# Attention banks laid out anew: products of 320 and 256 columns instead of 512 and 64, and one exponential per sign

## The chip, the core and the metric

The kernel runs on one core of a Trainium2 chip. The metric is the device time of one execution in microseconds (us). Of the core's engines five names occur below: PE is TensorE (its weight loads are listed as PEld), ACT is ScalarE, DVE is VectorE, POOL is GpSimd, and SP is the queue that issues most DMAs. PE writes its products to PSUM, which has banks of 512 float32 columns; the products of one instruction lie in one bank.

## What is computed

A linear attention with exponential features, then two feed-forward stages on its output. The change touches only the attention. In its terms (8 batches, 8 heads, 576 tokens, 64 values per head, 128 features):

```python
def phi(x):
    proj = np.einsum('bhsd,df->bhsf', x, w_phi)
    proj = proj - np.max(np.abs(proj), axis=-1, keepdims=True)
    return np.concatenate([np.exp(proj), np.exp(-proj)], axis=-1)
q_p, k_p = (phi(q), phi(k))
kv = np.einsum('bhsf,bhsd->bhfd', k_p, v)
z = np.sum(k_p, axis=2)
num = np.einsum('bhsf,bhfd->bhsd', q_p, kv)
den = np.einsum('bhsf,bhf->bhs', q_p, z)[..., None] + 1e-06
return (num / den).astype(np.float32)
```

The result x goes through a mixing with the previous token, products with w_k, w_v and w_r (stage 1, `y_scr` in HBM holds its result), and then through w_in, a convolution over 3 tokens, a gate and w_out (stage 2).

## The kernel before

**Staging.** `phase_1` does the attention and stage 1 of all 8 batches, `phase_2` does stage 2. In `phase_1` the attention of batch 0 runs first and alone (`first_attention_steps`), while the weights of stage 1 are loaded, rounded by ACT and their remainders taken by POOL (L560). After that, each `iteration(c)` mixes stage 1 of batch c with the attention of batch c+1: `fill` puts tiles of stage 1 (K, R, V; 288 columns each) between the steps of the attention, by the costs in `PE_NS` and `FILL_NS`. These lists give every engine its order; semaphores join the engines. Within an engine nothing overtakes in the program.

**Attention of one pair of heads.** Two heads share the 128 partitions: head 0 has rows 0 to 63 of q and k, head 1 has rows 64 to 127. There are 4 pairs in a batch, 32 in all. The steps of a pair, by their names in the lists:

- E (`features_and_keys`, L597): the tail of the keys (`k_tail`, 128 columns, all 128 rows), the features of the queries (`feature_chunk`, the products q_in,phi) and 8 tiles of keys (`key_tile`). Batch 0 has F (`features_only`, L618) and G (`keys_only`) in its place. Products of head 0 use the upper 64 rows of the array, those of head 1 the lower 64, and PE runs the two beside each other.
- QT (`part_maxima`): DVE turns the features of both heads (`q_turn`, L974) and takes maxima (`q_part`); M: PE turns the maxima, DVE spreads them (`max_blocks`).
- KV, then PICK: PE sums keys times values, then `subtract_maxima` adds the negative maxima onto the features (max_blocks,pick), and `turn_back` (L692) turns the sums that ACT has copied out (`kvt`, L850). ACT then takes the exponentials (`exp_q`, L843), with `copy_back` of the sums after the first of them.
- DEN (`sum_den`, one row per head and sign; `sum_den_wide` for two pairs of batch 0) and NUM (`attend`): the products q_exp,kvz. ACT copies both results out, and the denominators go through HBM.

**The banks.** The 576 columns of a head don't fit in a bank. `att_psum` gives the three banks. Before, head 0 begins at column 0: 512 of its columns lie in bank 0 and 64 in bank 1. Head 1 begins at column 960: 64 columns lie in bank 1 and 512 in bank 2. The tail of the keys and the turned maxima lie between them in bank 1. `CHUNKS` holds these pieces and each product of queries is made piece by piece. Three products of different rows of the array write to bank 1, so the semaphore `shared_bank` keeps them apart: each waits until the one before it has ended.

## Time and profile before

| what | value |
|---|---|
| median of 3 runs | 1280.31 us (1279.93 to 1280.62) |
| the profiled execution | 1280.67 us, of which its span is 1278.9 us |
| PE busy | 1261.5 us, 99% of the span |
| DVE busy | 825.9 us, 65% |
| ACT busy | 553.5 us, 43% |
| POOL busy | 142.9 us, 11% |
| granted clock of PE | 0.999 over the span (2.4 GHz) |

The profile shows one execution. Its span runs from the first to the last instruction; 1.8 us of the execution lie around it. Products overlap in PE's pipeline, so the durations of single products are longer than the time that each adds: what one adds is read from the distance of its start to the next start. A float32 product is listed as two instructions with one weight load each, called passes below; the rounded ones (xy_hi, max_blocks and the like) are one.

### The profile page before, as it was taken

What the parts mean: (1) busy time and instruction counts of PE and PEld (TensorE: products, weight loads), DVE (VectorE), ACT (ScalarE), POOL (GpSimd) and SP (SyncE); (2) the same over time, 40 slices, a digit from 0 to 9 for tenths busy, and PEclk for the clock granted to TensorE, in tenths of its full rate; (3) what the DMA queues carried; (4) which work ended last, traced back from release to release, by engine and by line L of the source; (5) the groups of instructions that cost most, each with busy time, mean ns of one, the idle gap of its engine ahead of it and who ended that gap; (6) DMA issues with size and microseconds to landing.
All of it is one profiled execution on the core that took longest, in us unless ns stands there. A gap on an engine that the chain in (4) does not pass through costs nothing.

```text
span 1278.9 us, 23739 instructions
## 1 busy us (share of the span) xinstructions
PE 1261.5 (99%) x9548; PEld 1081.1 (85%) x9548; DVE 825.9 (65%) x1350; ACT 553.5 (43%) x1059; POOL 142.9 (11%) x137
## 2 busy tenths in 40 slices
PE   8899999999999999999999999999999999999998
PEld 6678797888788878888788878999889898898997
DVE  7888666676476666757656666546584593673863
ACT  4653543535435354353442544454343352352441
POOL 3412111211111211121111211000000000000000
PEclk9999999999999999999999999999999999999999
DMA  6512222221312212221131120421102102022001
GB/s 185 170 31 65 56 59 66 57 65 40 89 40 60 74 46 59 74 63 51 41 89 49 51 79 17 146 63 59 70 1 79 57 15 78 1 71 79 1 34 42
DMA packets 91700, 79.03 MB, mean 62 GB/s; under 512 B 61896, under 2 KB 70472, under 8 KB 90568
## 3 DMA queue, kind: packets, MB, share of 16 engines
q1 hardware_dynamic: 91432, 77.46, 20.0%
q8 instruction: 76, 1.25, 0.4%
q14 instruction: 32, 0.26, 0.1%
q10 hardware_dynamic: 160, 0.07, 0.0%
HBM read 58.21 MB, written 19.01 MB: 60 GB/s over the span
## 4 chain that ended last, share of the span: by engine, by line
PE 89%; DVE 4%; issue 3%; DMA 2%; ACT 2%; SPq 0%; ACTq 0%; DVEq 0%
PE psm L580 36%; PE ps L580 20%; PE psh L1221 6%; PE psh L1222 6%; PE psh L1220 6%; PE pso L1222 5%; PE pso L1221 5%; PE pso L1220 5%; DMA den<-den_scr 1%; ACT k_signs L832 1%; DMA den_scr<-den_cols 1%; PE ps L692 1%; DVE q_turn L974 1%; DVE q_part L977 0%; DMA phi<-in_w_phi 0%
## 5 line engine op out<-in xcount | busy, mean ns | idle before, releaser
L580 PE MATMUL psm<-xy_hi,wk_hi 128*128 128x288 f32 x512 | 156.5, 306 | 4.9 <-ACT relu L884 3.2
L580 PE MATMUL psm<-k_hi,wv_hi 128*128 128x288 f32 x512 | 153.8, 300 | 0.0
L1222 PE MATMUL psh<-xy_hi,win_lo 128*128 128x288 f32 x512 | 151.3, 296 | 0.0
L1220 PE MATMUL psh<-xy_hi,win_hi 128*128 128x288 f32 x512 | 151.3, 296 | 0.0
L1221 PE MATMUL psh<-xy_lo,win_hi 128*128 128x288 f32 x512 | 151.3, 296 | 0.0
L580 PE MATMUL psm<-xy_lo,wk_hi 128*128 128x288 f32 x512 | 151.1, 295 | 0.0
L580 PE MATMUL psm<-k_lo,wv_hi 128*128 128x288 f32 x512 | 150.9, 295 | 0.0
L580 PE MATMUL psm<-k_hi,wv_lo 128*128 128x288 f32 x512 | 150.8, 295 | 0.0
L580 PE MATMUL psm<-xy_hi,wk_lo 128*128 128x288 f32 x512 | 150.7, 294 | 0.0
L568 POOL TENSOR_TENSOR z_pairs<-k_signs 128x512 f32<-128x512 f32 x56 | 73.2, 1306 | 601.0 <-ACT k_signs L832 597.0
L1066 DVE TENSOR_TENSOR k_lo<-square,k_hi 128x288 fp32r<-128x288 f32 x128 | 76.6, 620 | 63.8 <-ACT square L889 63.0
L832 ACT ACTIVATE k_signs<-k_signs 128x1152 f32<-128x1152 f32 x32 | 37.2, 1163 | 156.0 <-issue 140.0
L580 PEld LDWEIGHTS psm<-xy_hi,wk_hi 128*128 128x128 f32 x512 | 96.1, 188 | 9.5 <-ACT relu L884 5.4
L1222 PE MATMUL pso<-wk_hi,g_lo 128*128 128x512 f32 x256 | 101.3, 396 | 0.0
L1220 PE MATMUL pso<-wk_hi,g_hi 128*128 128x512 f32 x256 | 101.3, 396 | 0.0
L1221 PE MATMUL pso<-wk_lo,g_hi 128*128 128x512 f32 x256 | 101.2, 395 | 0.0
L580 PE MATMUL ps<-q_exp,kvz 128*64 128x512 f32 (+2 forms) x960 | 98.4, 409 | 0.0
L580 PEld LDWEIGHTS psm<-k_hi,wv_hi 128*128 128x128 f32 x512 | 96.2, 188 | 1.8
L1221 PEld LDWEIGHTS psh<-xy_lo,win_hi 128*128 128x128 f32 x512 | 96.3, 188 | 0.3
L1220 PEld LDWEIGHTS psh<-xy_hi,win_hi 128*128 128x128 f32 x512 | 96.2, 188 | 0.3
L580 PEld LDWEIGHTS psm<-xy_lo,wk_hi 128*128 128x128 f32 x512 | 96.3, 188 | 0.0
L580 PEld LDWEIGHTS psm<-xy_hi,wk_lo 128*128 128x128 f32 x512 | 96.3, 188 | 0.0
(151 smaller groups left out, 2791.3 us busy)
## 6 DMA issues: line engine op xcount, KB each, us to landing
k_in<-in_k SPq DMA_DIRECT2D x32, 320.0 KB, 3.3
v_nat<-in_v SPq DMA_DIRECT2D x32, 320.0 KB, 3.5
q_in<-in_q SPq DMA_DIRECT2D x32, 288.0 KB, 3.1
y_scr<-y SPq DMA_DIRECT2D x64, 144.0 KB, 2.4
y<-y_scr SPq DMA_DIRECT2D x8, 1152.0 KB, 5.6
den<-den_scr SPq DMA_DIRECT2D x60, 144.0 KB, 3.0
out<-rows SPq DMA_DIRECT2D x32, 256.0 KB, 2.0
stage<-in_moe_w_in SPq DMA_DIRECT2D x4, 512.0 KB, 3.9
```

What stands on the lines that cost most here:

```text
L568: nc.gpsimd.tensor_tensor(z_pairs[:], tiles[:, 0], tiles[:, 1], ALU.add).then_inc(z_paired, 1)
L580: return nc.tensor.matmul(o, lhsT, rhs, start=first, stop=last, skip_group_check=True)
L692: last = nc.tensor.matmul(sums_back()[:, i, :], kvt[:, i, :], ident[:], start=True, stop=True, is_transpose=True, skip_group_check=True)
L832: nc.scalar.activation(k_exp, k_shift, ACT.Exp).then_inc(k_exp_ready, 1)
L974: nc.vector.transpose(q_turn[:, h, :], q_cols(h, p, a)).then_inc(q_turned, 1)
L1066: nc.vector.tensor_tensor(k2_lo[:, i, :], square[:, i % 2, :], k2_hi[:, i, :].bitcast(F32), ALU.subtract).then_inc(k2_lo_ready, 1)
L1220: nc.tensor.matmul(o, wh, xh, start=first, stop=False, skip_group_check=True)
L1221: nc.tensor.matmul(o, wh, xl, start=False, stop=False, skip_group_check=True)
L1222: return nc.tensor.matmul(o, wl, xh, start=False, stop=last, skip_group_check=True)
```

## The change

The two heads lie side by side, from column 192 to column 1344 of the three banks. Head 0 has 320 columns in bank 0 and 256 in bank 1, head 1 has 256 in bank 1 and 320 in bank 2. The tail of the keys moves to the front of bank 0, and the turned maxima behind head 1. The bytes computed are the same; every piece of 512 or 64 columns becomes one of 320 or 256.

Since both heads are now one stretch of 1152 columns, `exp_q` takes one exponential for each sign (2 of 1152 columns for 4 of 576), and `part_maxima` has one turn of 1152 columns for 2 of 576. `q_exp_ready` counts 2 for each pair instead of 4.

E and F now share `project_queries`: tail of the keys, then the bank 2 piece of head 1 and the bank 1 piece of head 0, then the bank 0 piece of head 0, then the bank 1 piece of head 1. In E the 8 tiles of keys all follow behind; before, three of them stood between the pieces.

```diff
-    Q0, K_TAIL, Q_MAX, Q1 = 0, BANK + D, BANK + D + 2 * F, 2 * BANK - D
-    CHUNKS = (((0, BANK), (BANK, S)), ((0, D), (D, S)))
+    HEAD_PART = BANK // 2
+    K_TAIL, Q0, Q1, Q_MAX = 0, BANK + HEAD_PART - S, BANK + HEAD_PART, BANK + HEAD_PART + S
+    CHUNKS = (((0, S - HEAD_PART), (S - HEAD_PART, S)), ((0, HEAD_PART), (HEAD_PART, S)))
...
+    def both_heads(p, a):
+        return att_psum(p, a)[:, Q0:Q0 + 2 * S].rearrange("p (h s) -> p h s", h=2)
...
+        def project_queries(p, a):
+
+            mm(k_tail(p, a), k_in[:, p % 2, P * (TT - 1):P * TT], phi[:], True, True).then_inc(shared_bank, 1)
+            feature_chunk(p, a, 1, 1, True)
+            feature_chunk(p, a, 0, 1, True).then_inc(shared_bank, 1)
+            await_(pe, shared_bank, 2 * PAIRS, a, 2 * p + 1)
+            feature_chunk(p, a, 0, 0, True)
+            await_(pe, shared_bank, 2 * PAIRS, a, 2 * p + 2)
+            feature_chunk(p, a, 1, 0, False).then_inc(raw_features, 1)
...
-            mm(k_tail(p, a), k_in[:, p % 2, P * (TT - 1):P * TT], phi[:], True, True).then_inc(shared_bank, 1)
-            feature_chunk(p, a, 1, 1, True)
-            feature_chunk(p, a, 0, 0, True)
-            key_tile(p, 1, 0)
-            await_(pe, shared_bank, 2 * PAIRS, a, 2 * p + 1)
-            feature_chunk(p, a, 0, 1, True).then_inc(shared_bank, 1)
-            key_tile(p, 1, 1)
-            key_tile(p, 0, 0)
-            await_(pe, shared_bank, 2 * PAIRS, a, 2 * p + 2)
-            feature_chunk(p, a, 1, 0, False).then_inc(raw_features, 1)
-            for h, t in ((0, 1), (1, 2), (0, 2), (1, 3), (0, 3)):
-                last = key_tile(p, h, t)
+            project_queries(p, a)
+            for t in range(TT - 1):
+                for h in (0, 1):
+                    last = key_tile(p, h, t)
...
-            for h in range(2):
-                for e in range(2):
-                    nc.scalar.activation(q_exp[:, e, h, :], q_cols(h, p, a), ACT.Exp, scale=1.0 - 2.0 * e).then_inc(q_exp_ready, 1)
-                    if a and h == e == 0:
-                        copy_back(p, a)
+            for e in range(2):
+                nc.scalar.activation(q_exp[:, e, :, :], both_heads(p, a), ACT.Exp, scale=1.0 - 2.0 * e).then_inc(q_exp_ready, 1)
+                if a and e == 0:
+                    copy_back(p, a)
...
-            for h in range(2):
-                nc.vector.transpose(q_turn[:, h, :], q_cols(h, p, a)).then_inc(q_turned, 1)
+            nc.vector.transpose(q_turn[:].rearrange("p h s -> p (h s)"), att_psum(p, a)[:, Q0:Q0 + 2 * S]).then_inc(q_turned, 1)
```

PE, the step E of a pair in the mixed iterations. In the program's order before (ps<-q_in,phi are the features, ps<-phi,k_in of the first row is the tail of the keys, the others are tiles of keys):

```order
L580 MATMUL ps<-phi,k_in 128x128 [waits q_loaded0,z_copied,k_loaded0,kvz_copied,num_copied]
L580 MATMUL ps<-q_in,phi 128x512 x2
L580 MATMUL ps<-phi,k_in 128x128
L580 MATMUL ps<-q_in,phi 128x64 [waits shared_bank]
L580 MATMUL ps<-phi,k_in 128x128 x2
L580 MATMUL ps<-q_in,phi 128x64 [waits shared_bank]
L580 MATMUL ps<-phi,k_in 128x128 x5
```

And now:

```order
L584 MATMUL ps<-phi,k_in 128x128 [waits q_loaded0,z_copied,k_loaded0,kvz_copied,num_copied]
L584 MATMUL ps<-q_in,phi 128x320
L584 MATMUL ps<-q_in,phi 128x256
L584 MATMUL ps<-q_in,phi 128x320 [waits shared_bank]
L584 MATMUL ps<-q_in,phi 128x256 [waits shared_bank]
L584 MATMUL ps<-phi,k_in 128x128 x8
```

The three tiles of keys that stood ahead of the last wait for `shared_bank` have moved behind it; one product of 320 columns stands there instead.

ACT, the step PICK of a pair in the mixed iterations, before:

```order
L850 ACTIVATE kvt<-ps 128x384 [waits kv_turned,kv_summed]
L843 ACTIVATE q_exp<-ps 128x576 [waits attended,features]
L855 ACTIVATE kvz<-ps 128x4x64 [waits attended,kv_turned]
L856 ACTIVATE kvz<-ps 128x4
L843 ACTIVATE q_exp<-ps 128x576 x3
L884 ACTIVATE relu<-psm 128x288 [waits k_squared,k_done]
```

And now:

```order
L849 ACTIVATE kvt<-ps 128x384 [waits kv_turned,kv_summed]
L842 ACTIVATE q_exp<-ps 128x1152 [waits attended,features]
L854 ACTIVATE kvz<-ps 128x4x64 [waits attended,kv_turned]
L855 ACTIVATE kvz<-ps 128x4
L842 ACTIVATE q_exp<-ps 128x1152
L883 ACTIVATE relu<-psm 128x288 [waits k_squared,k_done]
```

The copies of the sums (kvz) stand behind an exponential of 1152 columns instead of one of 576, and one exponential instead of three stands behind them. Nothing else changes its place.

## Rows read from the trace of the kernel before

**Rows 1.** The page: the span, and the chain that ended last by engine.
```profile
span 1278.9 us, 23739 instructions
...
PE 89%; DVE 4%; issue 3%; DMA 2%; ACT 2%; SPq 0%; ACTq 0%; DVEq 0%
```

**Rows 2.** Busy us (xinstructions) per engine: batch 0's attention, then the mixed iterations.
```profile
0.00:67.20 67.20, 57.59 (x454) 41.69 (x454) 53.02 (x77) 35.17 (x50) 26.27 (x25) 1.00 0.56 169
67.20:808.00 740.80, 736.72 (x6216) 610.83 (x6217) 487.59 (x851) 328.19 (x701) 116.62 (x112) 1.00 0.21 58
```

**Rows 3.** Timeline (start us, us, engine), step E of one pair, PE.
```profile
619.82 0.33 PE L580 MATMUL ps<-q_in,phi 64*128 64x64 f32 x2
...
620.27 0.32 PE L580 MATMUL ps<-q_in,phi 64*128 64x64 f32 x1
```

**Rows 4.** Timeline, the same step E, PE's weight loads.
```profile
618.85 0.30 PEld L580 LDWEIGHTS ps<-q_in,phi 64*128 64x128 f32 x4
...
620.26 0.18 PEld L580 LDWEIGHTS ps<-q_in,phi 64*128 64x128 f32 x1
...
620.37 0.19 PEld L580 LDWEIGHTS ps<-q_in,phi 64*128 64x128 f32 x1
...
621.13 0.19 PEld L580 LDWEIGHTS psm<-xy_hi,wr_hi 128*128 128x128 f32 x1
```

**Rows 5.** Timeline, a step F of batch 0, PE's weight loads.
```profile
28.92 0.30 PEld L580 LDWEIGHTS ps<-q_in,phi 64*128 64x128 f32 x4
29.46 0.19 PEld L580 LDWEIGHTS ps<-q_in,phi 64*128 64x128 f32 x1 [0.24 <-issue]
29.89 0.19 PEld L580 LDWEIGHTS ps<-q_in,phi 64*128 64x128 f32 x1 [0.24 <-issue]
30.27 0.29 PEld L580 LDWEIGHTS ps<-q_in,phi 64*128 64x128 f32 x2 [0.19 <-PE ps L580]
30.63 0.41 PEld L580 LDWEIGHTS ps<-v_nat,k_signs 128*128 128x128 f32 x3
```

**Rows 6.** Timeline, step PICK of one pair, PE's weight loads.
```profile
609.26 0.64 PEld L580 LDWEIGHTS ps<-max_blocks,pick 128*128 128x128 f32 x4 [0.22 <-issue]
609.95 0.36 PEld L692 LDWEIGHTS ps<-ident,kvt 128*128 128x128 f32 x3
```

**Rows 7.** Timeline, step PICK of another pair, PE's weight loads.
```profile
105.19 0.64 PEld L580 LDWEIGHTS ps<-max_blocks,pick 128*128 128x128 f32 x4 [0.72 <-DVE max_blocks L993]
105.77 0.46 PEld L692 LDWEIGHTS ps<-ident,kvt 128*128 128x128 f32 x3
```

**Rows 8.** Timeline, ACT in the step PICK of Rows 6.
```profile
609.40 0.49 ACT L850 ACTIVATE kvt<-ps 128x384 f32<-128x384 f32 x1 [1.67 <-PE ps L580]
...
611.12 1.76 ACT L843 ACTIVATE q_exp<-ps 128x576 f32<-128x576 f32 x3
612.72 0.47 ACT L884 ACTIVATE relu<-psm 128x288 f32<-128x288 f32 x1
```

**Rows 9.** Timeline, ACT, an exponential of 1152 columns of the keys.
```profile
599.80 1.17 ACT L836 ACTIVATE k_signs<-k_signs 128x1152 f32<-128x1152 f32 x1
600.88 0.39 ACT L884 ACTIVATE relu<-psm 128x288 f32<-128x288 f32 x1
```

**Rows 10.** Timeline, steps DEN and NUM of one pair, PE's weight loads.
```profile
613.67 0.22 PEld L580 LDWEIGHTS ps<-q_exp,kvz 128*1 128x1 f32 x16 [0.17 <-issue]
...
616.52 0.26 PEld L580 LDWEIGHTS ps<-q_exp,kvz 128*64 128x64 f32 x6 [0.28 <-issue]
616.85 0.19 PEld L580 LDWEIGHTS psm<-xy_hi,wr_hi 128*128 128x128 f32 x1
```

**Rows 11.** Timeline, DVE, both turns of one pair.
```profile
598.44 1.44 DVE L974 STREAM_TRANSPOSE q_turn<-ps 128x576 f32<-128x576 f32 x2
```

**Rows 12.** Timeline of batch 0's attention, DVE.
```profile
32.22 1.35 DVE L977 TENSOR_REDUCE q_part<-q_turn 128x36 f32<-128x1152 f32 x1
33.61 0.85 DVE L981 COPY q_part<-q_part 128x64 f32<-128x64 f32 x1
```

**Rows 13.** The same stretch, POOL.
```profile
31.99 2.42 POOL L560 TENSOR_TENSOR wv_lo<-mix,wv_hi 128x1024 fp32r<-128x1024 f32 x1
```

**Rows 14.** Timeline, PE, the first tile of stage 1.
```profile
67.28 0.37 PE L580 MATMUL psm<-xy_hi,wk_hi 128*128 128x288 f32 x1 [1.20 <-DVE xy_lo L1061]
```

More of the change, by code:

```diff
@@ L622, in features_only @@
             await_(pe, k_loaded[p % 2], 16 * (PAIRS // 2), a, 16 * (p // 2 + 1))
-            mm(k_tail(p, a), k_in[:, p % 2, P * (TT - 1):P * TT], phi[:], True, True).then_inc(shared_bank, 1)
-            feature_chunk(p, a, 1, 1, True)
-            feature_chunk(p, a, 0, 0, True)
-            await_(pe, shared_bank, 2 * PAIRS, a, 2 * p + 1)
-            feature_chunk(p, a, 0, 1, True).then_inc(shared_bank, 1)
-            await_(pe, shared_bank, 2 * PAIRS, a, 2 * p + 2)
-            feature_chunk(p, a, 1, 0, False).then_inc(raw_features, 1)
+            project_queries(p, a)
         def keys_only(p, a):
@@ L699, in sum_den @@
             await_(pe, z_copied, PAIRS, a - 1, p + 1)
-            await_(pe, q_exp_ready, 4 * PAIRS, a, 4 * p + 4)
+            await_(pe, q_exp_ready, 2 * PAIRS, a, 2 * p + 2)
             for chunk in CHUNKS[1]:
@@ L710, in sum_den_wide @@
             await_(pe, kvz_copied, PAIRS, a, p + 1)
-            await_(pe, q_exp_ready, 4 * PAIRS, a, 4 * p + 4)
+            await_(pe, q_exp_ready, 2 * PAIRS, a, 2 * p + 2)
             for chunk in CHUNKS[1]:
@@ L972, in part_maxima @@
             await_(dve, raw_features, PAIRS, a, p + 1)
-            for h in range(2):
-                nc.vector.transpose(q_turn[:, h, :], q_cols(h, p, a)).then_inc(q_turned, 1)
-            await_(dve, q_turned, 2 * PAIRS, a, 2 * p + 2)
+            nc.vector.transpose(q_turn[:].rearrange("p h s -> p (h s)"), att_psum(p, a)[:, Q0:Q0 + 2 * S]).then_inc(q_turned, 1)
+            await_(dve, q_turned, PAIRS, a, p + 1)
             await_(dve, max_turned, PAIRS, a, p)
```

## The prediction, made before the changed kernel was run

> **What bounds the kernel now.** I read the page first: the chain that ended last is PE for 89% of the span [rows 1]. Then the busy times by stretch [rows 2]. In the mixed iterations, 67.2 to 808 us, PE is busy 736.72 of 740.80 us, while DVE has 253 us of idle time, ACT 413 and POOL 624. Only the attention of batch 0 is different: PE is busy 57.59 of 67.20 us and DVE 53.02, so a chain through several engines sets the end there. In the mixed iterations, therefore, only what PE itself does in its order counts, and a faster DVE or ACT brings nothing unless PE waits for it. In batch 0 the latency of a pair counts. Stage 2 is not touched. Last I read PE's order in the three steps that the change touches, in the distances of starts. I looked at all pairs: the distances agree within 0.01 us, so one pair stands for all 28 mixed pairs (where one doesn't, I say so). All of it runs at the full granted clock, as the fields 1.00 of both stretches show.
>
> **Step E, features and keys.** From the first load of the queries (618.85) to the load of the next tile (621.13) it takes 2.28 us [rows 4]. Each half of the array (one head each) has its own work. A pass of 512 columns takes 0.43 us, the distance of two loads (29.46, 29.89) that each wait for the start of such a pass [rows 5]; I take other sizes in proportion, 0.27 for 320 and 0.21 for 256. A pass can't be shorter than a weight load, whose distance is 0.11 (620.26, 620.37) [rows 4], so a pass of 64 columns after a wait costs 0.11, and so does one of 128. Before, a half does 2 x 0.43, 2 x 0.11 and 8 x 0.11. After, it does 2 x 0.27, 2 x 0.21 and 8 x 0.11: 0.96 for 1.08, 0.12 less. But the wait has moved. The last piece (head 1, bank 1) waits until head 0's piece in bank 1 has ended. How long this takes is in step F: there the second pass of the short piece loads at 0.97 (29.89), is loaded at 1.08 and streamed at 1.13, and the waiting piece loads at 1.35 (30.27) [rows 5]: 0.22 from the last column to the release. Before, in E, tiles of keys ran in both halves during this wait. After, only one product of head 0 does, and head 1's half stands empty. The sum: head 1's first piece has streamed at 0.11 + 2 x 0.27 = 0.65, head 0's bank 1 piece at 0.11 + 2 x 0.21 = 0.53 to 0.54, so the last piece loads at 0.76, streams from 0.87 to 1.30, and 8 passes of keys follow to 2.18 or 2.19. With the change-over to a full array, 0.09 or 0.10 (1.13 + 0.11 to 30.63 leaves no more than that in F), the next tile loads at 2.28. Before: 2.28. **The shorter passes are lost to the wait; E costs 0.00 us.** The bounds are -0.03 and the rivals below. The features are ready some 0.4 us sooner than before (the last piece loads at 0.76, not 1.41), but DVE's large maxima still need the last tile of keys, which ends when it did.
>
> **Step PICK.** Four rounded products. After the first load, the fifth load (turn_back's) comes at 0.69 (609.26 to 609.95) [rows 6], and its product 0.11 later, at 0.80. Two of the four have 64 columns and cost a load of 0.11 each; that is where 256 columns would be free. The products before are 0.11 + 0.22 + 0.11 + 0.11 + 0.22 = 0.77; now 0.11 + 0.14 + 0.12 + 0.12 + 0.14 = 0.63 (a rounded product takes half a float32 pass and some 0.01). That would be 0.14 less. But the fifth load waits for ACT's copy `kvt`, which ends at 609.40 + 0.49 = 609.89, 0.06 ahead of the load [rows 8]. That copy hangs on the step KV ahead of PICK and doesn't move. Where PICK itself came late, the fifth load came at 0.58 [rows 7]: there alone, once in 28 pairs, the copy covers nothing. **So 27 pairs gain 0.00 us, one gains 0.14.**
>
> **Steps DEN and NUM.** 3.18 us (613.67 to 616.85) [rows 10]. The loads here are short (1 or 64 columns), so 64-column passes are nearly as good as others: the last four steps of 64 columns and the change-over take 616.52 to 616.85, 0.33; without 0.09 for the change-over that is 0.06 a step, against 0.053 in proportion. The new pieces save this excess: **0.02 us a pair**.
>
> **ACT and DVE.** Three exponentials of 576 columns take 611.12 to 612.72, 0.53 us each [rows 8]; one of 1152 takes 599.80 to 600.88, 1.08 [rows 9]. Four times 0.53 is 2.13, twice 1.08 is 2.16: the merging brings nothing. The two new exponentials read PSUM, the row reads SBUF, so I keep 0.1 us on both sides. The copies kvz come 0.5 us later; DEN, which needs them, begins at 613.67 [rows 10], 0.95 us after ACT has gone on to its next tile at 612.72 [rows 8], so they stay hidden. DVE's two turns last 1.44 us together [rows 11]; a reduction of 1152 elements lasts 1.35 [rows 12], my value for one turn of as many: 0.1 less, hidden by DVE's idle time in the mixed iterations.
>
> The Trainium skill (ScalarE: Activation LUTs, What ACT_TABLE_LOAD costs) gives an ACTIVATE 186 ns and 0.833 ns for each element, of which 93 ns overlap. By that, four of 576 would take 2.29 us and two of 1152 2.11, 0.19 less for each pair; over the four pairs of batch 0 at most 0.8 us less. The rows of this case show 2.13 and 2.16, and I go by them.
>
> **Batch 0.** Each pair's chain has one turn (0.1 less) and one PICK (0.14 less, since no turn_back follows). Step F falls from 1.71 (28.92 to 30.63) [rows 5] to 1.40, 0.3 less. If all four pairs kept all of this, 4 x 0.24 + 0.3 = 1.3 us would go. But POOL takes much of it back: DVE's copy at 33.61, some 0.2 us long at its shortest, lasted 0.85 [rows 12] and ended with POOL's instruction, 31.99 + 2.42 = 34.41 [rows 13]. If DVE comes sooner, it waits longer for POOL. I followed the chain to the first tile, for which PE stands idle 1.20 us [rows 14], shifting each start: two of the pairs end in such a wait and keep 0.1, and 0.3 us is left at the end. Bounds: 1.3 less, and 0.5 more (a long DVE instruction that newly falls under one of POOL).
>
> **The sum**, against the profiled execution, 1280.67 us (span 1278.9 and 1.8 around it): 28 x (0.00 + 0.00 - 0.02) = -0.56, the one PICK -0.14, batch 0 -0.3: -1.0 us, 1279.7. The median of the runs is 0.36 lower than the profiled execution, so the forecast is **1279.3 us**, -0.08%. Its own bounds: 28 x -0.03 and the rest of batch 0 give 1277.5, no gain and 0.5 more in batch 0 give 1280.8.
>
> **Rivals.**
>
> *The release comes in order (17%).* Head 0's bank 1 piece follows head 1's bank 2 piece in the order. If its end counts only once the longer one has ended (0.65 and not 0.54), the last piece loads 0.10 later: 28 x 0.10 = 2.8 us, 1282.1. For it: in E the waiting load came at 1.41, in F at 1.35, though the short piece streamed at the same time; something beside that piece delayed it by 0.06. Against: in the earlier layout the orders of the two halves were always of the same length, so no row shows whether one half waits for the other. The Trainium skill (TensorE: Matmul & The Clock Gate, The mechanism) says that matmuls start and end in program order without exception; by this rule the time would be this rival's.
>
> *The slower side: the waiting load needs an empty array (15%).* In E before, the short piece's passes are listed until 619.82 + 0.33 = 620.15, and the waiting piece begins at 620.27 [rows 3], just when the tiles of keys in flight in both halves had ended. If that is the rule after a wait, the last piece can load only when head 0's bank 0 piece has streamed, at 0.54 + 2 x 0.27 = 1.08 and not at 0.76. Head 1's half then stands empty 0.32 us longer, on PE's own path in each of 28 pairs: +9.0 us, 1288.3. It outweighs all gains (1.0 us) as soon as the load is 0.04 us late. Against it: turn_back's load at 609.95 waited for ACT too and came while the last product of PICK, until about 610.03, was still streaming [rows 6].
>
> *PICK's gain survives (5%).* If the fifth load is set by something that moves with the products, 27 x 0.13 = 3.6 us go: 1275.7. Against it speaks that it came 0.10 sooner where the copy was early [rows 7].
>
> *Nothing moves (9%).* DVE meets POOL as before at each point of batch 0, and E rounds up: 1280.3.
>
> **Chances and range.** The forecast has 54%. The range 1277.5 to 1283.1 holds it, the release in order with its bounds, and the case in which nothing moves; it leaves out 20%. About 0.2% (2.6 us) is what a measurement of this kernel can tell from no change. Faster by more: PICK's gain (5%) and the lower edge of the forecast (3%), 8%. Slower by more: the empty array (15%) and the upper edge of the release in order (3%), 18%. Within: 74%.
>
> **What would show it.** E from the first load of the queries to the next tile: 2.28 (2.38 and 2.60 under the rivals), with the last piece's load at 0.76 (0.86, 1.08). PICK's fifth load at 0.69 after the first, with a gap ahead of it that was not there. DEN and NUM 3.16. Two exponentials at 1.08 each. The first tile of stage 1 at 67.0. I would be wrong if PE's stream in a half depended on the other half, or if DVE's turn of 1152 columns were slower than two of 576.

## The result, and the profile after

The changed kernel takes **1281.53 us** (median of 20 runs, 1280.16 to 1284.75) against 1279.32 us (20 runs, 1278.39 to 1282.03) for the kernel before: a ratio of 1.0017, 95% interval 1.0012 to 1.0023. It is 2.2 us slower, where 1.0 us less was forecast. (The forecast of 1279.3 was reckoned from a median of 3 runs, 1280.31; over 20 runs the kernel before has 1279.32.) Among the runs of bank1_first, bank1_first_key_ahead and m_late_warm, below, is one execution each of 1.7 to 4.3 ms; without it their medians move by less than 0.3 us. The profiled execution took 1282.21 us with a span of 1280.4 us.

The page has hardly moved: PE still carries 89% of the chain that ended last [rows 1].

```profile
span 1280.4 us, 23643 instructions
...
PE 89%; DVE 4%; issue 3%; ACT 2%; DMA 2%; POOL 0%; SPq 0%; ACTq 0%; DVEq 0%
```

Step E, PE's weight loads (start us, us), three stretches of the same pair as in [rows 4]: the first load, the loads around the last piece (620.25 to 621.12), and the next tile.

```profile
620.25 0.19 PEld L584 LDWEIGHTS ps<-q_in,phi 64*128 64x128 f32 x2
...
621.12 0.18 PEld L584 LDWEIGHTS ps<-q_in,phi 64*128 64x128 f32 x1
621.13 0.18 PEld L584 LDWEIGHTS ps<-phi,k_in 64*128 64x128 f32 x1
...
622.64 0.19 PEld L584 LDWEIGHTS psm<-xy_hi,wr_hi 128*128 128x128 f32 x1
```

E takes 2.39 us (620.25 to 622.64) for 2.28 before. Its last piece loads 0.87 or 0.88 after the first load; 0.76 was forecast. All 28 mixed pairs agree within 0.01 us.

PICK of the pair in [rows 6], PE's weight loads:

```profile
610.72 0.56 PEld L584 LDWEIGHTS ps<-max_blocks,pick 128*128 128x128 f32 x4 [0.22 <-issue]
611.40 0.31 PEld L692 LDWEIGHTS ps<-ident,kvt 128*128 128x128 f32 x3
611.68 0.19 PEld L584 LDWEIGHTS psm<-xy_hi,wk_hi 128*128 128x128 f32 x1
```

The fifth load comes 0.68 after the first, as before. But turn_back then lasts 0.28 us to the next tile (611.40 to 611.68), where it lasted 0.33 (609.95 to 610.28; the next tile before):

```profile
610.28 0.19 PEld L580 LDWEIGHTS psm<-xy_hi,wk_hi 128*128 128x128 f32 x1
```

ACT in the same step [rows 8], with the two long exponentials, 1.03 and 1.02 us from start to the next start:

```profile
610.86 0.49 ACT L849 ACTIVATE kvt<-ps 128x384 f32<-128x384 f32 x1 [1.67 <-PE ps L584]
611.55 1.13 ACT L842 ACTIVATE q_exp<-ps 128x1152 f32<-128x1152 f32 x1 [0.20 <-PE ps L584]
612.58 0.38 ACT L854 ACTIVATE kvz<-ps 128x256 f32<-128x256 f32 x1
...
612.89 1.15 ACT L842 ACTIVATE q_exp<-ps 128x1152 f32<-128x1152 f32 x1
613.91 0.44 ACT L883 ACTIVATE relu<-psm 128x288 f32<-128x288 f32 x1
```

DVE's one turn of 1152 columns starts at 599.91, and the reduction behind it at 601.31:

```profile
599.91 1.37 DVE L972 STREAM_TRANSPOSE q_turn<-ps 128x1152 f32<-128x1152 f32 x1
601.31 1.35 DVE L975 TENSOR_REDUCE q_part<-q_turn 128x36 f32<-128x1152 f32 x1
```

In batch 0, step F of [rows 5] takes 1.50 us (28.34 to 29.84) for 1.71:

```profile
28.34 1.17 PEld L584 LDWEIGHTS ps<-q_in,phi 64*128 64x128 f32 x8
29.84 0.30 PEld L584 LDWEIGHTS ps<-v_nat,k_signs 128*128 128x128 f32 x2 [0.33 <-issue]
```

And there the granted clock is not whole any more. Three stretches of batch 0 (us, PE busy, granted clock, DMA share, GB/s), and PE ahead of M of pair 3:

```profile
46.00:49.00 3.00, 0.58 (x9) 1.00 0.89 233
49.00:52.00 3.00, 3.00 (x17) 0.62 0.24 59
52.00:55.00 3.00, 3.00 (x21) 0.81 0.80 272
```

```profile
48.81 0.30 PE L646 MATMUL psm<-ident,q_part 128*128 128x128 f32 x1 [2.42 <-DVE k_signs L958]
```

PE was idle for 2.42 us, and then part of the next stretches ran at the lower level, 1.2 GHz. In the profile of before the clock is 1.00 throughout batch 0. The first tile of stage 1 starts at 68.14 us; it was 67.28 [rows 14]. Whether the clock costs this time is looked at under batch 0, below.

Where the 2.2 us are, by the traces: from the first E of the mixed iterations (91.29 before, 91.77 after) to the end of the span, stage 2 included, it takes 1187.6 us before and 1188.6 after. Two further traces of the same kernels (below) give 1187.4 and 1188.9. So some 1.2 us are lost in the mixed iterations, and about 1 us is left for batch 0. That rest is a difference of medians less a difference of traces: the first E alone differs by 1.5 us between two traces of one kernel (below).

### The profile page after: what moved, and what is told of

It reads as the page before. It is cut to its first block, busy times and chain, and to the rows that moved or that the text cites. A ratio compares the mean times of both kernels' runs of the same rounds, so it can differ in the third digit from the quotient of the medians.

```text
span 1280.4 us, 23643 instructions
## 1 busy us (share of the span) xinstructions
PE 1262.1 (99%) x9548; PEld 1098.6 (86%) x9548; DVE 825.7 (64%) x1318; ACT 551.2 (43%) x995; POOL 143.0 (11%) x137
## 4 chain that ended last, share of the span: by engine, by line
PE 89%; DVE 4%; issue 3%; ACT 2%; DMA 2%; POOL 0%; SPq 0%; ACTq 0%; DVEq 0%
PE psm L584 36%; PE ps L584 20%; PE psh L1219 6%; PE psh L1220 6%; PE psh L1218 6%; PE pso L1219 5%; PE pso L1218 5%; PE pso L1220 5%; PE ps L692 1%; ACT k_signs L832 1%; DVE q_turn L972 1%; DMA den<-den_scr 1%; DVE q_part L975 1%; DMA den_scr<-den_cols 1%; DMA phi<-in_w_phi 0%
## 5 line engine op out<-in xcount | busy, mean ns | idle before, releaser
L584 PE MATMUL ps<-q_exp,kvz 128*64 128x320 f32 (+2 forms) x960 | 99.8, 413 | 0.0
L584 PEld LDWEIGHTS psm<-k_lo,wv_hi 128*128 128x128 f32 x512 | 96.3, 188 | 0.0
```

What stands on the lines that cost most here:

```text
L584: return nc.tensor.matmul(o, lhsT, rhs, start=first, stop=last, skip_group_check=True)
```

## The experiments

Each kernel was timed beside the kernel before on the same chip, but not all on one chip: the groups can be told by the column "before" (1279.79, 1279.30, 1279.61, 1279.03). Between groups, compare the differences from the kernel before. Medians in us, E and the load of its last piece in us after the first load:

| kernel | median (lowest run, runs) | before | ratio (95%) | E | last piece |
|---|---|---|---|---|---|
| bank1_first | 1277.25 (1276.25, 12) | 1279.79 | 0.9982 (0.9968 to 0.9996) | 2.27 | 0.75 |
| bank1_first_key_ahead | 1271.50 (1270.77, 6) | 1279.79 | 0.9929 (0.9909 to 0.9950) | 2.06 | 0.76 |
| m_late | 1281.13 (1279.58, 12) | 1279.79 | 1.0009 (0.9995 to 1.0022) | 2.39 | 0.88 |
| layout_alone | 1280.98 (1280.17, 12) | 1279.79 | 1.0006 (0.9995 to 1.0017) | 2.39 | 0.88 |
| before_again | 1279.48 (1278.40, 11) | 1279.30 | 1.0003 (0.9994 to 1.0012) | 2.28 | 1.42 |
| after_again | 1281.55 (1280.12, 11) | 1279.30 | 1.0014 (1.0005 to 1.0023) | 2.39 | 0.88 |
| pick_extra | 1282.20 (1281.22, 9) | 1279.30 | 1.0027 (1.0018 to 1.0037) | 2.39 | 0.88 |
| keys_behind | 1290.18 (1288.88, 4) | 1279.30 | 1.0084 (1.0070 to 1.0098) | 2.66 | 1.35 |
| key_ahead | 1275.90 (1275.22, 9) | 1279.61 | 0.9965 (0.9950 to 0.9981) | 2.17 | 0.88 |
| all_best | 1271.15 (1270.86, 5) | 1279.61 | 0.9936 (0.9924 to 0.9948) | 2.06 | 0.76 |
| round_in_parts | 1282.29 (1280.24, 12) | 1279.61 | 1.0021 (1.0010 to 1.0032) | 2.39 | 0.88 |
| m_late_warm | 1279.99 (1278.74, 11) | 1279.03 | 1.0008 (0.9999 to 1.0017) | 2.39 | 0.88 |
| all_best_warm | 1273.43 (1270.02, 5) | 1279.03 | 0.9944 (0.9931 to 0.9958) | 2.06 | 0.76 |

### Step E: what releases the last piece

**bank1_first**: head 0's bank 1 piece goes ahead of head 1's longer one; nothing else moves.

```diff
+            feature_chunk(p, a, 0, 1, True).then_inc(shared_bank, 1)
             feature_chunk(p, a, 1, 1, True)
-            feature_chunk(p, a, 0, 1, True).then_inc(shared_bank, 1)
```

> The changed kernel with one exchange: head 0's piece in bank 1 is issued ahead of head 1's piece in bank 2. In the changed kernel the last piece of a step E loads 0.88 us after the first load, and E takes 2.39 us. Theory A, the release comes in the order of the products (the short piece counts as ended only when the longer one issued ahead of it has ended): now nothing longer is ahead of it, so the last piece loads at 0.76 to 0.78 and E takes 2.28 to 2.29; 29 steps x 0.10 = 2.9 us less than the changed kernel. Rival B, the last piece can load only when its own half of the array has drained (head 1's first piece, which takes as long as before): the load stays at 0.86 to 0.88 and E at 2.38 to 2.39, the time unchanged. Rival C, both halves must be empty: excluded already by 0.88, which lies ahead of the end of head 0's bank 0 piece at 1.07.

PE's weight loads, step E of the same pair: first load, last piece, next tile.

```profile
615.73 0.94 PEld L584 LDWEIGHTS ps<-q_in,phi 64*128 64x128 f32 x7
...
616.48 0.18 PEld L584 LDWEIGHTS ps<-q_in,phi 64*128 64x128 f32 x1
...
618.00 0.19 PEld L584 LDWEIGHTS psm<-xy_hi,wr_hi 128*128 128x128 f32 x1
```

The last piece loads at 0.75 instead of 0.88 and E is 2.27. The same products in the same halves, only their order differs: the release of the bank 1 piece had waited for the longer product issued ahead of it in the other half of the array. That this wait needs an empty half is refuted. The kernel is 4.3 us faster than the changed one (2.5 below its before, where the changed kernel is 2.2 above): 28 x 0.123 = 3.4 of it is E, the rest was not followed up.

**bank1_first_key_ahead** also puts one tile of keys of head 1 ahead of the last wait, so that head 1's half has work during it. **key_ahead** does this alone, without the exchange.

```diff
-        def project_queries(p, a):
+        def project_queries(p, a, ahead=()):
...
             feature_chunk(p, a, 0, 0, True)
+            for h, t in ahead:
+                key_tile(p, h, t)
             await_(pe, shared_bank, 2 * PAIRS, a, 2 * p + 2)
...
-            project_queries(p, a)
-            for t in range(TT - 1):
-                for h in (0, 1):
-                    last = key_tile(p, h, t)
+            project_queries(p, a, ((1, 0),))
+            for h, t in ((0, 0), (1, 1), (0, 1), (1, 2), (0, 2), (1, 3), (0, 3)):
+                last = key_tile(p, h, t)
```

> As bank1_first, and one tile of keys of head 1 (two passes of 0.11) stands ahead of the last wait, so that head 1's half has work until 0.86. If what E loses is the empty half of the array and nothing else (theory A and B alike), the passes now follow each other: 0.11 + 0.54 + 0.22 + 0.43 + 6 x 0.11 = 1.96, with the change-over 2.06 us for E against 2.39 in the changed kernel and 2.29 in the one before. That is 28 x 0.33 = 9 us less than the changed kernel and 28 x 0.27 = 7.5 us less than the kernel before with the gain in the step PICK: a ratio to the kernel before of about 0.994. If the shorter passes were no gain at all (rival: a pass of 256 or 320 columns costs more than in proportion), E would stay at 2.17 or more.

> The changed kernel with one tile of keys of head 1 ahead of the last wait of E; the order of the two short pieces stays as in the changed kernel. It tells whether the late release costs by itself or only because head 1's half stands empty during it. Theory one (the release comes in order, at 0.88 after the first load, and PE loses only what nothing fills): the last piece loads at 0.88 to 0.89, the tile's two passes lie ahead of it at 0.65 and 0.76, and E falls by two passes of 0.11 from 2.39 to 2.18; 28 x 0.21 = 6.0 us less than the changed kernel, 1275.5 us. Theory two (the tile ahead of the wait pushes the waiting piece back by its own length): last piece at 1.0 or later, E 2.3 to 2.4, 1279 to 1281.5 us.

With key_ahead the release is as late as in the changed kernel (0.88), but E falls by 0.22: two passes of 0.11 now lie under the wait. PE's weight loads: the first load, the last piece with a load of the other half beside it, and the next tile:

```profile
198.93 0.52 PEld L584 LDWEIGHTS ps<-q_in,phi 64*128 64x128 f32 x5
...
199.81 0.18 PEld L584 LDWEIGHTS ps<-q_in,phi 64*128 64x128 f32 x1
199.81 0.18 PEld L584 LDWEIGHTS ps<-phi,k_in 64*128 64x128 f32 x1
...
201.10 0.19 PEld L584 LDWEIGHTS psm<-xy_hi,wr_hi 128*128 128x128 f32 x1
```

So the late release costs only what stands empty meanwhile. 28 x 0.223 = 6.2 us were to go; 6.0 went (2.25 above its before in after_again, 3.71 below in key_ahead). Both cures together bring E to 2.06 and the kernel to 1271.50 us, as expected: 8.3 us below the kernel before.

**keys_behind** asks the same of the old layout: the kernel before with its three covering tiles moved behind the waits.

```diff
-            key_tile(p, 1, 0)
             await_(pe, shared_bank, 2 * PAIRS, a, 2 * p + 1)
             feature_chunk(p, a, 0, 1, True).then_inc(shared_bank, 1)
-            key_tile(p, 1, 1)
-            key_tile(p, 0, 0)
             await_(pe, shared_bank, 2 * PAIRS, a, 2 * p + 2)
             feature_chunk(p, a, 1, 0, False).then_inc(raw_features, 1)
-            for h, t in ((0, 1), (1, 2), (0, 2), (1, 3), (0, 3)):
+            for h, t in ((1, 0), (0, 0), (1, 1), (0, 1), (1, 2), (0, 2), (1, 3), (0, 3)):
```

> The kernel before, in its old layout with pieces of 512 and 64 columns, but with all 8 tiles of keys behind the last wait in E, as the changed kernel has them. It takes the cover of the wait away and leaves all lengths. Theory one (three tiles of keys filled the wait): E is then step F with 8 tiles behind it: the last piece loads at 1.35 after the first as in F, its two passes take 0.11 each, 8 passes of keys in each half 0.88, and the change-over 0.10: 2.55 instead of 2.28, 28 x 0.27 = 7.5 us more than before, 1287.1 us. Theory two (PE is bound by its total of passes in a half and the wait costs nothing wherever it stands): E stays at 2.28 and the time at 1279.6 us.

The last piece loads at 1.35, as in F, but E is 2.66 and not 2.55, because the expectation left out the 0.11 us in which the waiting piece's own weights are loaded into an empty half. 28 x 0.377 = 10.6 us; measured 10.7 (1290.18 less 1279.48). Without cover E takes 2.66 in the old layout and 2.39 in the new one: the new lengths save 0.27 and the cover of the old order was worth 0.38. This run also bears on the release: with no tile of keys issued ahead of the short piece, the last piece loads at 1.35 and not at 1.42.

### PICK: does ACT's copy cover it

**pick_extra** repeats one product of 256 columns in PICK.

```diff
-            for h in range(2):
-                for chunk in CHUNKS[h]:
+            for h, chunks in enumerate((CHUNKS[0], (CHUNKS[1][:1] if a else ()) + CHUNKS[1])):
+                for chunk in chunks:
```

> The changed kernel with one more product of 256 columns in PICK of the 28 mixed pairs (head 1's bank 1 piece has its maxima subtracted twice, so the output is another). It measures what cover ACT's copy of the sums gives. Theory one (the load of turn_back waits for that copy, as predicted): the fifth load of PICK stays at 0.68 after the first where PICK has PE waiting for the copy; where the copy is early it comes 0.12 to 0.14 later than 0.51. Turn_back follows products that have only just ended and gets back to 0.33 from 0.28, so a pair costs 0.05 to 0.08, 28 pairs 1.4 to 2.2 us, 1283.3 us. Theory two (the load is set by the products): it moves to 0.80, and the kernel takes 28 x 0.13 = 3.6 us longer, 1285.1 us.

PE's weight loads in one PICK:

```profile
187.90 0.68 PEld L584 LDWEIGHTS ps<-max_blocks,pick 128*128 128x128 f32 x5 [0.23 <-issue]
188.58 0.32 PEld L692 LDWEIGHTS ps<-ident,kvt 128*128 128x128 f32 x3
188.87 0.19 PEld L584 LDWEIGHTS psm<-xy_hi,wk_hi 128*128 128x128 f32 x1
```

With five products turn_back's load still comes at 0.68: the copy sets it, as predicted. But turn_back stays at 0.29, so the extra product costs 0.65 us in all (1282.20 less 1281.55), where 1.4 to 2.2 were expected; the traces show 0.01 in each of 27 pairs and 0.11 in the one that the copy doesn't cover. Turn_back is thus not slowed by how much ran ahead of it. What fits all three traces is that it waits for a product that is still streaming: its first product is listed 0.11 after its load before, where the last old product has 512 columns (610.06 after 609.95), and 0.07 after it here (188.65 after 188.58), where that has 320.

### The mergers on ACT and DVE

**layout_alone** keeps the new layout with four exponentials and two turns (q_exp_ready still counts 2).

```diff
-            for e in range(2):
-                nc.scalar.activation(q_exp[:, e, :, :], both_heads(p, a), ACT.Exp, scale=1.0 - 2.0 * e).then_inc(q_exp_ready, 1)
+            for h in range(2):
+                for e in range(2):
+                    done = nc.scalar.activation(q_exp[:, e, h, :], q_cols(h, p, a), ACT.Exp, scale=1.0 - 2.0 * e)
...
-            nc.vector.transpose(q_turn[:].rearrange("p h s -> p (h s)"), att_psum(p, a)[:, Q0:Q0 + 2 * S]).then_inc(q_turned, 1)
+            for h in range(2):
+                nc.vector.transpose(q_turn[:, h, :], q_cols(h, p, a)).then_inc(q_turned, 1)
```

> The changed kernel with both mergers undone: four exponentials of 576 columns and two turns of 576, in the new layout of the banks. If the mergers bring nothing in the mixed iterations (my step), all distances on PE from 90 us on stay as in the changed kernel within 0.01 us: E 2.39, PICK to turn_back 0.68, DEN and NUM 3.17, and an iteration of 105.5 us. In batch 0 each pair is 0.1 to 0.25 us slower. The time lies within 1 us of the changed kernel. Rival: the mergers are what slows it (the copies kvz come 0.5 us later behind the longer exponential); then this kernel is faster than the changed one by 1 us or more.

In the mixed iterations nothing differs (E 2.39, PICK 0.68, DEN and NUM 3.17), and the medians 1280.98 and 1281.53 can't be told apart by their intervals. ACT there:

```profile
611.64 1.76 ACT L843 ACTIVATE q_exp<-ps 128x576 f32<-128x576 f32 x3
613.23 0.47 ACT L886 ACTIVATE relu<-psm 128x288 f32<-128x288 f32 x1
```

The last three take 0.53 each, and the first took 0.55: 2.14 us against 2.05 of the merged ones. The 0.09 are hidden.

### Batch 0: meetings and the granted clock

**before_again** and **after_again** are the two kernels once more.

> The kernel before, unchanged, run once more to see how much of batch 0 differs from execution to execution. In the trace at hand its granted clock stays at 1.00 through batch 0, and the first step E of the mixed iterations begins at 91.29 us. Theory one (the changed kernel loses about 1 us in batch 0 because PE's longer idle stretch there brings the half clock): the clock stays at full here again, E of the first mixed pair begins at 91.3 +-0.2, and the median is 1279.3 to 1279.8 us. Theory two (the clock falls somewhere in batch 0 in any of the kernels, by chance of the execution): a stretch at half clock shows here too, and E begins later than 91.3 by up to 1.7 us.

> The changed kernel, unchanged, run once more beside the kernel before on the same chip. In the mixed iterations nothing should differ from its first trace: E 2.39, the fifth load of PICK at 0.68 and turn_back 0.28, so 1.0 us over the whole of them. Theory one (half clock behind the idle 2.42 us ahead of M of pair 3): again a stretch at half clock near 50 us, and the first mixed E at 91.8. Theory two (chance): the stretch lies elsewhere, has another length or is not there, and the first mixed E begins between 90.3 and 91.8; the median is then 1.0 to 2.2 us above before whichever it is. Median expected: 1281.5 +-0.5 us.

before_again keeps the full clock in batch 0; its first mixed E starts at 89.83, where theory one said 91.3: executions of one kernel differ by 1.5 us here. In after_again that E starts at 90.82, and the half clock lies elsewhere, behind an idle time of 0.94 us of PE ahead of M of pair 0, which was 0.52 in the kernel before. Rows of PE, busy and clock:

```profile
15.00:18.00 3.00, 2.87 (x20) 0.77 0.00 0
18.00:21.00 3.00, 3.00 (x21) 0.66 0.49 117
```

The mean granted clock that each run lists says how often this is so. Runs at 1.000: 77 of 101 for the kernel before, 7 of 31 for the changed kernel. Theory two has the place right (it varies), theory one the tendency. Two limits. A mean of 0.999 need not come from batch 0: the kernel before shows it in both its traces with a full clock there, because the clock also falls at the very end (us; busy us of PE, PEld, DVE, ACT and POOL; clock; DMA share; GB/s):

```profile
67.20:1270.00 1202.80, 1198.56 (x9050) 1034.24 (x9051) 772.47 (x1274) 517.54 (x1008) 116.62 (x112) 1.00 0.18 55
1270.00:1278.90 8.90, 5.36 (x46) 5.16 (x44) 0.41 (x1) 0.77 (x2) 0.00 (x0) 0.92 0.35 113
```

And the changed kernel's 7 runs at 1.000 have a median of 1281.16 us, its other 24 of 1281.77, while the 77 of the kernel before have 1279.41. So 1.75 of the 2.2 us are there at full clock too. That leaves some 0.5 us for the clock (an estimate, from 7 runs) and, of the about 1 us of batch 0, about as much for something else.

The old layout is not free of the fall either: in the trace of keys_behind PE idles 2.12 us ahead of M of pair 3, and the clock is at its lower level from 49.8 to 53.2.

**m_late** puts M of pair 3 behind NUM of pair 2 on PE in batch 0.

```diff
             if m is None:
+                late = ("M", PAIRS - 1)
+                steps = [s for s in steps if s != late]
+                steps.insert(steps.index(("NUM", PAIRS - 2)) + 1, late)
```

> The changed kernel with one exchange in PE's order in the attention of batch 0: the step M of pair 3 stands behind the steps DEN and NUM of pair 2, so that PE, which idled 2.4 us ahead of that M and then ran at the half clock for 3.4 us (DEN and NUM of pair 2 took 5.7 us and not 4.0), idles 1 us at most there. Theory D, a part of the slowdown is this fall of the clock: no half clock in the first 90 us, DEN and NUM of pair 2 at 4.0 to 4.1 us, the first tile of stage 1 about 1.5 to 2 us earlier than the 68.1 of the changed kernel, and the time 1 to 2 us below the changed kernel. Rival: the clock falls in few executions only and the slowdown lies in step E alone; then the time changes by less than 0.5 us.

The half clock near 50 us is gone (1.00 from 49 to 55), but one stands from 17 to 21 (0.86 for 15 to 18, 0.57 for 18 to 21). The median is 1.34 us above its before, where the changed kernel is 2.2 above: the intervals of the two ratios overlap.

**round_in_parts** splits one rounding of ACT into 8 instructions, to let POOL begin later.

```diff
-            nc.scalar.activation(hi[:, i:i + rows, :].rearrange("p r n -> p (r n)"), stage[n % 3], ACT.Copy).then_inc(piece_hi, 1)
+            parts = 8 if n == 6 else 1
+            for j in range(parts):
+                cols = slice(1024 // parts * j, 1024 // parts * (j + 1))
+                nc.scalar.activation(hi[:, i:i + rows, :].rearrange("p r n -> p (r n)")[:, cols], stage[n % 3][:, cols], ACT.Copy).then_inc(piece_hi, 1)
...
-            pool.wait_ge(piece_hi, n + 1)
+            pool.wait_ge(piece_hi, n + 1 + 7 * (n >= 6))
```

> The changed kernel, with one rounding of ACT in batch 0 (the seventh piece of the weights, 1024 columns, done from 40.45 to 41.5 us) made in 8 instructions of 128 columns. That takes about 1 us longer and lets POOL begin its subtraction of this piece at about 42.6 us instead of 41.6. Nothing else changes. Theory one (batch 0 of the changed kernel loses time because DVE's multiplication x of 576 columns, at 42.07 us, meets this subtraction of POOL and lasts 2.5 to 2.9 us instead of 0.76): x comes ahead of POOL and lasts 0.76, the turn of pair 3 begins at about 43 and not 44.5 to 44.9, and from PICK's end of pair 2 to the first tile of stage 1 it takes 20.5 us as in the traces with a short x, not 21.3 to 22.9; the median falls by 0.5 to 1.5 us to 1280.0 to 1281.0. Theory two (the meeting is hidden or comes back at the next subtraction): x is short but the first tile is no earlier, and the median stays at 1281.5 us.

DVE's x is short (0.76 for 2.48) and M comes 2.83 us after the tiles of G of pair 3 begin, for 3.55. But x starts 1.38 us later (43.45 for 42.07), so the turn behind it gains nothing (44.50 for 44.48), and the copy after it now meets POOL's next instruction (46.63 to 49.01). The copy in the changed kernel, and here:

```profile
47.27 0.20 DVE L979 COPY q_part<-q_part 128x64 f32<-128x64 f32 x1
```

```profile
47.31 1.75 DVE L982 COPY q_part<-q_part 128x64 f32<-128x64 f32 x1
```

Theory two holds: the meeting came back. The clock falls twice, near 17 and 50 us, and the median is not lower. So this run doesn't tell what the meeting costs the changed kernel. It is not new there either: in the trace of before the same x, at 42.93, lasts 2.71. (The 8 instructions may themselves delay what follows on ACT; that was not separated.)

**m_late_warm** fills the idle time ahead of M of pair 0 as well, with products that nobody reads.

```diff
-    steps = [("G", 0), ("F", 0), ("EK", 0), ("F", 1), ("QT", 0), ("WARM", 0), ("KV0", 0), ("M", 0)] + hi()
+    steps = [("G", 0), ("F", 0), ("EK", 0), ("F", 1), ("QT", 0), ("WARM", 0), ("KV0", 0), ("WARM", 0), ("M", 0)] + hi()
```

> The kernel with the late M (the changed kernel, M of pair 3 behind NUM of pair 2 in batch 0) and 4 more products of the identity on PE ahead of M of pair 0, where PE of the changed kernels stands idle for 0.91 to 1.14 us in place of 0.52 us, since step F got shorter. They take about 1.0 us. Theory one (the half clock of 15 to 23 us, seen with the new layout in 7 of 10 traces, follows on that longer idle time, and the half clock near 50 us on the idle time ahead of M of pair 3, which the late M removes): the granted clock is 1.00 in all stretches of batch 0, PICK of pair 0 begins 3.9 us after M of pair 0 at most instead of 4.2 to 5.3, and the median falls by 0.5 to 1.5 us from the late M's 1281.13, to 1279.6 to 1280.6: batch 0's share of the loss was the clock. Theory two (the clock falls by chance, or batch 0 waits for DVE and POOL anyway): a half clock shows again, or it doesn't and the median stays at 1281.1 +-0.4 us.

Granted clock where it had fallen (us, PE busy, clock, DMA share, GB/s):

```profile
15.00:18.00 3.00, 2.97 (x27) 1.00 0.00 0
18.00:21.00 3.00, 2.36 (x25) 1.00 0.71 171
49.00:52.00 3.00, 2.72 (x21) 1.00 0.06 6
```

9 runs of 10 are at 1.000 (m_late: 1 of 12; the kernel before, beside them, 14 of 15 and 22 of 29). The products do keep the clock up there. What this is worth in time is not shown: the median is 1.1 us below that of m_late, but the two ran in different groups, on different chips. Each against its own before, m_late is 1.34 us above and m_late_warm 0.96, with ratios of 1.0009 and 1.0008, which can't be told apart.

The profiled execution is the tenth run, of 1283.20 us, and speaks against the clock as the only cause: it has the full clock to 68 us and the first tile no earlier than 68.08. DVE's x of pair 1 (55.47) starts 0.04 us behind POOL's instruction, PE idles 3.76 us ahead of the first tile, and there the clock falls (DVE, then PE, then the stretch, in the fields given above):

```profile
55.47 2.98 DVE L1010 TENSOR_TENSOR x<-square,den 128x576 f32<-128x576 f32 x1 [2.19 <-DMA den<-den_scr]
```

```profile
68.08 0.49 PE L584 MATMUL psm<-xy_hi,wk_hi 128*128 128x288 f32 x1 [3.76 <-DVE xy_lo L1063]
```

```profile
67.00:70.00 3.00, 1.92 (x8) 1.95 (x9) 2.97 (x3) 0.00 (x0) 0.00 (x0) 0.70 0.00 0
```

**all_best** is bank1_first_key_ahead with the late M, **all_best_warm** adds the four products.

> The changed kernel with both cures of E (head 0's bank 1 piece issued first, one tile of keys of head 1 ahead of the last wait) and, in batch 0, the turn of the maxima of pair 3 behind NUM of pair 2 on PE. In the mixed iterations all should be as with the two cures alone: E 2.06, last piece loaded at 0.76, fifth load of PICK at 0.68. Theory one (the late M saves PE's idle time ahead of DEN in batch 0): the stretch from PICK of pair 2 in batch 0 to the first tile of stage 1 is 0.2 to 0.8 us shorter than with the cures alone, 1271.0 us. Theory two (batch 0 ends with DVE and POOL wherever M stands): 1271.5 us, no difference.

> The kernel with both cures of E and the late M, with the same 4 products ahead of M of pair 0. Theory one: clock 1.00 through batch 0, and 0.3 to 1.0 us less than the 1271.15 us without them, 1270.1 to 1270.9. Theory two: 1271.15 +-0.3 us. E stays at 2.06 in the mixed iterations.

All_best is at 1271.15 us, which its runs can't tell from 1271.50. All_best_warm missed both theories: its median is 2.3 us higher and not lower. It has two groups: 1270.0 and 1271.2, both at a mean clock of 1.000, and three runs of 1273.4 to 1273.9, all below that. Five runs can't say whether the four products caused the slow group. Its profiled execution is of that group. There DVE's x of pair 1 meets POOL (DVE, then POOL):

```profile
54.54 3.00 DVE L1011 TENSOR_TENSOR x<-square,den 128x576 f32<-128x576 f32 x1 [1.55 <-DMA den<-den_scr]
```

```profile
54.54 2.39 POOL L564 TENSOR_TENSOR wr_lo<-diff,wr_hi 128x1024 fp32r<-128x1024 f32 x1 [4.20 <-ACT wr_hi L831]
```

In the profile of all_best the same instruction starts ahead of POOL's and is short:

```profile
54.45 0.76 DVE L1011 TENSOR_TENSOR x<-square,den 128x576 f32<-128x576 f32 x1 [0.50 <-DMA den<-den_scr]
```

The instruction itself takes 2.24 us more in the first case. Part of it comes back: in all_best the next x (57.10) meets the same POOL instruction and takes 1.10, for 0.46. The first tile starts at 67.17 and at 65.48, 1.69 apart. This x is long (2.98, 3.00) in the two traces with the four products and 0.76 in all 13 others. That the products bring the meeting about, by shifting what stands behind them, would fit; it was not tested.

## Why the prediction was wrong, step by step

- **What bounds the kernel** held: in every variant the loss or gain in the mixed iterations is that of PE's own order.
- **Step E** is the step that failed. It took the release to follow the end of head 0's piece in its own half (0.54) and so put the last piece at 0.76. It came at 0.88: 0.65, the end of the longer product issued ahead, and 0.23 from its last column to the release (0.22 was the prediction's value). E cost 0.107 x 28 = 3.0 us instead of nothing. This was the rival *the release comes in order* (0.86, 2.38, 2.8 us), and bank1_first shows it. The Trainium skill (TensorE: Matmul & The Clock Gate, The mechanism) says that matmuls start and end in program order; for the ends the runs agree, 0.88 in one order and 0.75 in the other. The listed starts of second passes don't follow the order here: head 0's piece 620.58, head 1's, issued ahead of it, 620.62. The rival's number for the whole, 1282.1, lies 0.6 above the measured median; with the kernel before at 1279.3 and not 1280.3 it would have been 1281.1, 0.4 below.

  The prediction held that no row could decide this, since the two halves had equal orders before. That was a misreading. In E before, a tile of keys of head 1 is issued ahead of head 0's short piece. The second passes of the two (PE, before: the short piece, the tile), and of head 1's longer product in the changed kernel:

```profile
619.87 0.27 PE L580 MATMUL ps<-q_in,phi 64*128 64x64 f32 x1
619.92 0.39 PE L580 MATMUL ps<-phi,k_in 64*128 64x128 f32 x3
```

```profile
620.62 0.60 PE L584 MATMUL ps<-q_in,phi 64*128 64x320 f32 x2
```

  The tile has streamed at 619.92 + 0.11 = 620.03 and the waiting load comes at 620.26 [rows 4], 0.23 later. After: 620.62 + 0.27 = 620.89, and the load at 621.12, 0.23 later as well. That is the 0.06 by which E's load was late against F (1.41 for 1.35), which the prediction had noted as "something beside that piece"; keys_behind takes the tile away and has 1.35.
- **The empty array** was refuted: last piece at 0.88, not 1.08.
- **PICK**: cover right, one term mis-sized. The fifth load stayed at 0.68. In the one uncovered pair it came 0.07 sooner (0.51 for 0.58) and turn_back took 0.08 less, 0.15 together, where 0.14 was forecast. But in the other pairs turn_back was taken to begin 0.11 after its load, at 0.80, behind the last old product, which streams until about 0.78. Its loads are shorter (grouped lines: mean 140 ns for ident,kvt, 188 for max_blocks,pick), so before it did wait for that product, and now it doesn't (its first product is listed 0.11 after its load before, and its second load follows the first by 0.06 now): 0.056 less in each of 27 pairs, -1.5 us, where 0.00 stood. The grouped lines, after:

```profile
L584 PEld LDWEIGHTS ps<-max_blocks,pick 128*128 128x128 f32 x120 | 16.8, 188 | 7.1 <-issue 6.4 <-DVE max_blocks L991 0.7
L692 PEld LDWEIGHTS ps<-ident,kvt 128*128 128x128 f32 x84 | 8.7, 140 | 3.3
```

- **DEN and NUM**: 3.172 for 3.180, 0.01 a pair for 0.02: -0.2 us for -0.56.
- **ACT and DVE**: right. Two exponentials of 1.03 and 1.02 (1.08 forecast, within the 0.1 kept), the turn at 1.40 from start to start (1.35 forecast), so it saved 0.04 and not 0.1; both hidden. The Trainium skill's figures (ScalarE: Activation LUTs, What ACT_TABLE_LOAD costs) made the gain 0.19 a pair; 0.09 was measured.
- **Batch 0**: wrong in sign, about +1 for -0.3. F fell to 1.50, not 1.40; the late release found in E (0.11) is as large as this miss. What it freed on PE became idle time ahead of M (0.91 for 0.52 in pair 0), DVE's chain being no faster, and this idle time was priced at nothing; the traces show the clock at 1.2 GHz behind it. By the medians of runs at full clock this is some 0.5 us; the cause of the other half stays open. The collision of DVE and POOL was seen as a mechanism, but it was bounded by 0.5 us, and one meeting lengthens an instruction by up to 2.24; that the changed kernel has more of them than the kernel before is not shown.
- **The sum**: 28 x (0.107 - 0.01), 27 x -0.056 and the one -0.15 give +1.1 in the mixed iterations (traces: +1.0 and +1.5). The about +1 of batch 0 is what is left of the measured +2.2, so it confirms nothing. The bound of the range (1283.1) held because it covered the rival; that two misses of opposite sign, PICK and batch 0, nearly cancelled is luck.

## What to carry to other kernels

A semaphore on a product counts when the products issued ahead of it have ended too, also those in the other half of the array: issue the product that others wait for first, and put work of the waiting half ahead of the wait. Equalising lengths saved less (0.27) than the cover it displaced (0.38). And engine time that a change frees ahead of a wait is not free of consequences: look at what the granted clock does behind the new idle time, over many runs and not in one profile, and compare the times of runs with and without the fall before you call it the cause.

## What the runs showed that I had not expected

- The release in program order across the halves: 0.88 or 0.75 for the same product, by its place alone.
- A product after a wait costs its own weight load (0.11) when its half is empty: 2.66 for 2.55.
- Small idle times of PE early in batch 0 went with the lower clock level: with 0.91 to 1.14 us ahead of M of pair 0 the clock falls near 17 us in 7 of 8 traces, with 0.50 to 0.52 (old layout) in none of 3. About 1.0 us of filling products brought the full clock back in 9 runs of 10. How much time that saves is not shown.
- A DVE instruction of 0.76 us takes up to 3.00 when it starts with or just behind one of POOL, and 0.76 when it starts 1.0 us ahead of it (54.45 and 55.49 in all_best).
- What stays open: what, beside the clock, costs the changed kernel about 0.5 us in batch 0; why the first loads of batch 0 shift by up to 2 us between executions; and whether the four products help at all, since both traces that have them show the long x.
